# Natural-order casts with parity copies, and Ln and Exp in two pieces, in a strided sparse attention with a rational MLP

## What is computed

```python
scores = scale * np.matmul(q, k.transpose(0, 1, 3, 2))
mask_local = (rel >= 0) & (rel < stride)
mask_strided = (rel >= 0) & (pos[None, :] % stride == pos[:, None] % stride)
...
attn = attn / (np.sum(attn, axis=-1, keepdims=True) + 1e-09)
...
h = x @ w_in
P = a[0] + a[1] * h + a[2] * h2 + a[3] * h3
Q = 1.0 + np.abs(b[0]) * np.abs(h) + np.abs(b[1]) * h2
g = P / (Q + 1e-06)
return (g @ w_out).astype(np.float32)
```

## Time and profile before

| what | value |
|---|---|
| three runs, median (lowest to highest) | 556.41 us (552.62 to 563.49) |
| the profiled execution, its own time | 551.65 us |
| its span, first to last instruction | 549.87 us |
| busy: TensorE, VectorE, ScalarE, POOL | 353.3, 345.4, 255.2, 95.9 us |
| DMA packets, bytes | 176,959, 60.35 MB |

### The profile page before, as it was taken

The page is one execution under the profiler, slowest core; times in us unless marked ns, Lnnn a source line. Parts: engine busy times, 40 slices in busy tenths (PEclk is TensorE's granted clock), DMA queues, the critical chain, the costliest instruction groups (busy, mean ns, idle before and its releaser), DMA issues.

```text
span 549.9 us, 7027 instructions
## 1 busy us (share of the span) xinstructions
PE 353.3 (64%) x2993; PEld 162.9 (30%) x3040; DVE 345.4 (63%) x286; ACT 255.2 (46%) x249; POOL 95.9 (17%) x104
## 2 busy tenths in 40 slices
PE   0010123355662996898479677999998769988763
PEld 0000112113221442444134333344443323333221
DVE  2000013012885795899449758799998996999920
ACT  0010001021735473666707516768847865788500
POOL 9400000050041061514301600010020110100100
PEclk9999999995955797998859967999999989999888
DMA  9999992799299999999994986442261211010101
GB/s 133 119 91 101 184 137 58 131 176 92 46 164 160 160 164 186 194 185 175 186 121 88 161 163 138 87 104 63 61 139 31 60 62 39 38 39 19 57 29 49
DMA packets 176959, 60.35 MB, mean 110 GB/s; under 512 B 164384, under 2 KB 173600, under 8 KB 176416
## 3 DMA queue, kind: packets, MB, share of 16 engines
q1 hardware_dynamic: 133088, 32.11, 40.9%
q0 software_dynamic: 43840, 27.79, 37.5%
HBM read 42.83 MB, written 25.95 MB: 125 GB/s over the span
## 4 chain that ended last, share of the span: by engine, by line
DVE 31%; PE 22%; DMA 16%; SPq 14%; ACT 10%; issue 5%; POOL 0%; DVEq 0%; POOLq 0%
PE ps_h L649 10%; DMA ptL<-pL 8%; PE ps_out L691 7%; SPq L433 6%; DVE u L668 6%; DVE z L676 4%; DMA xt<-xs 4%; SPq L442 4%; DMA xs<-xS 3%; DVE z L674 3%; DVE h L678 3%; ACT u L671 3%; DVE u L666 3%; ACT u L669 3%; DVE z L664 3%
## 5 line engine op out<-in xcount | busy, mean ns | idle before, releaser
L691 PE MATMUL ps_out<-Wout,h 128*128 128x512 bf16 x557 | 144.0, 410 | 24.5 <-ACT os L696 19.3
L649 PE MATMUL ps_h<-xt,Win 128*128 128x512 bf16 x548 | 137.7, 396 | 27.1 <-DMA xt<-xs 12.7
L653 ACT ACTIVATE h<-ps_h 128x512 bf16<-128x512 f32 x144 | 84.9, 597 | 79.8 <-PE ps_h L649 79.8
L691 PEld LDWEIGHTS ps_out<-Wout,h 128*128 128x128 bf16 x576 | 57.0, 104 | 101.5 <-ACT os L696 23.2
L649 PEld LDWEIGHTS ps_h<-xt,Win 128*128 128x128 bf16 x576 | 50.7, 101 | 96.5 <-ACT h L653 32.2
L702 POOL DMA_DIRECT2D out_dram<-os x36 | 37.1, 1121 | 241.1 <-ACT os L696 230.5
L669 ACT ACTIVATE u<-u,consts 128x4096 bf16<-128x4096 bf16 x18 | 66.7, 3706 | 17.2 <-DVE u L668 17.0
L389 POOL DMA_DIRECT2D lq<-in_q_dram x16 | 37.4, 2381 | 206.4 <-DMA vL<-v 205.6
L671 ACT ACTIVATE u<-u 128x4096 bf16<-128x4096 bf16 x18 | 65.1, 3619 | 0.0
L696 ACT ACTIVATE os<-ps_out 128x512 f32<-128x512 f32 x36 | 21.5, 597 | 62.3 <-PE ps_out L691 62.2
L389 POOL DMA_DIRECT2D lk<-in_k_dram x16 | 46.7, 3005 | 0.0
(11 more groups left out here) (41 smaller groups left out, 352.7 us busy)
## 6 DMA issues: line engine op xcount, KB each, us to landing
out_dram<-os POOLq DMA_DIRECT2D x36, 256.0 KB, 3.3
v<-in_v_dram POOLq DMA_DIRECT2D x8, 576.0 KB, 12.1
vL<-v SPq DMA_DIRECT2D x32, 96.0 KB, 3.3
lq<-in_q_dram POOLq DMA_DIRECT2D x16, 144.0 KB, 12.1
lk<-in_k_dram POOLq DMA_DIRECT2D x16, 144.0 KB, 13.5
sq<-in_q_dram POOLq DMA_DIRECT2D x8, 288.0 KB, 7.1
sk<-in_k_dram POOLq DMA_DIRECT2D x8, 288.0 KB, 9.6
vS<-v SPq DMA_DIRECT2D x16, 144.0 KB
```

Source lines behind the costliest of these rows:

```text
L649: r = e.matmul(ph.t[:, :], Win[:, kk, f * 128:(f + 1) * 128], xt.t[:, kk, :], start=(kk == 0), stop=(kk == NK1 - 1))
L653: P.op("act", lambda e, f=f, ph=ph, h=h: e.activation(h.t[:, f % G, :], ph.t[:, :], AF.Copy), 0.53, key, r=[ph], w=[h])
L691: r = e.matmul(po.t[:, :], groups[g].t[:, j, m * 128:(m + 1) * 128], Wout[:, kk, :], start=(kk == 0), stop=(kk == NF - 1))
```

## The change

1. Casts: q and k of all heads, and v of the local heads, go as they lie, in five issues of four heads each; nothing writes 128-byte runs any more. vS is cast by POOL straight from v in DRAM.
2. Loads: q and k come through four transposes, each of four heads and 1,152 rows (local first), all with even positions on the lower half of the partitions and odd ones on the upper. For the local heads four copies from SBUF to SBUF bring the odd positions of heads 0 and 1 to the lower half, and the even positions of heads 2 and 3 to the upper half. The halves of a tile have names of their own for the waits.
3. The local steps take heads 0 and 2, then 1 and 3, in the order local, strided, strided, local. A local score is 36 matmuls of 32 queries (one parity) where it was 18 of 64; the query rows of a block of 64 come out with even positions first, and a matmul writes its 96 columns as two interleaved sets of 48.
4. That order of rows holds through xL, xS and xt. The xs store writes runs of 2,048 numbers in that order. The h copy puts the columns back into their natural order as it writes.
5. Ln and Exp are issued in two pieces of 2,048 columns each, Ln, Ln, Exp, Exp, each waiting for the one before.
6. The last chunk's four sums use the attention's two PSUM tiles, four banks, in place of the one-bank ring.
7. Batch 1's casts and Wout wait for batch 0's loads (the last of vL, the local k); the casts of batch b+2 are written down after attention b. Planner: loads' key -700 becomes -20 (batch 0 keeps it), chunk c's becomes 512 c + 1500 (1000 for the first), mlp2's 1900 becomes 2250, some costs are new, and a DMA counts twice when another queue is busy.

```diff
-    R_lqT = ring("lqT", 4, [128, S])
...
+    SC = S // 2
+    SW = HL * SC
+    PRE = 2 * SC
+    QW = 2 * PRE + 2 * SW
+    R_tq = ring("tq", 2, [128, QW])
+    R_tk = ring("tk", 2, [128, QW])
...
+    def planes(j, idx):
+        if j == 0:
+            return PRE + idx * SC, PRE + SW * 2 + idx * SC
+        return idx * SC, PRE + (2 + idx) * SC
...
+        for n in range(2):
+            for s_t, d_t, t in ((q, q16, T_q[b][n]), (k, k16, T_k[b][n])):
+                bulk(s_t, d_t, b, HL * n, HL, H, t, key, after)
+            if n == 0:
+                bulk(v, vs, b, 0, HL, HL, T_v[b], key, after)
+        vS = vS_of[b] = R_vS.next()
+        for x in range(2):
+            P.op("pool", lambda e, x=x: e.dma_start(
+                vS.t[64 * x:64 * x + SB, :, :, :].rearrange("t h g d -> t h (g d)"),
+                bass.AP(tensor=v.tensor, offset=v.offset + ((b * H + HL) * S + 8 * x) * D,
+                        ap=[[16 * D, SB], [S * D, HL], [1, 8 * D]])),
+                1.0, key, w=[vS], dma=0.6, after=after)
...
+                P.op("sp", lambda e, t=t, d_t=d_t, n=n: e.dma_start_transpose(
+                    t.t[:, PRE + n * SW:PRE + n * SW + SW],
+                    d_t[b, HL * n:HL * n + HL, :, :].rearrange("h (c two) d -> (h c) (two d)", two=2)),
+                    1.3, key + 2 * n, r=[dt_], w=[hf], dma=1.5)
...
+                d0 = 0 if x else PRE + 2 * SW
+                s0 = 2 * PRE if x else PRE
+                P.op("sp", lambda e, t=t, x=x, d0=d0, s0=s0: e.dma_start(
+                    t.t[64 * x:64 * x + 64, d0:d0 + PRE], t.t[64 - 64 * x:128 - 64 * x, s0:s0 + PRE]),
+                    0.5, key + 1, r=[halves[t.name][0]], w=[z], dma=0.3)
...
-        for kind, idx in (("L", 0), ("S", 0), ("L", 2), ("S", 2)):
+        for kind, idx in (("L", 0), ("S", 0), ("S", 2), ("L", 1)):
...
+                        for qp in range(2):
+                            p0 = 64 * (jj % 2) + 32 * qp
+                            for j in range(2):
+                                even, odd = planes(j, idx)
+                                off = 64 * j * QW
+                                r = e.matmul(pst[p0:p0 + 32, j, KW * (jj // 2):KW * (jj // 2) + KW].rearrange(
+                                                 "p (c k) -> p k c", k=2),
...
-                bass.AP(tensor=xs, offset=(b * S + par) * 256, ap=[[16 * 256, SB], [2 * 256, NBK], [1, 256]]),
+                bass.AP(tensor=xs, offset=(b * S + 32 * par) * 256, ap=[[64 * 256, SB // 4], [8 * 256, 4], [1, 8 * 256]]),
...
-                P.op("act", lambda e, f=f, ph=ph, h=h: e.activation(h.t[:, f % G, :], ph.t[:, :], AF.Copy),
+                P.op("act", lambda e, f=f, ph=ph, h=h: e.activation(
+                    h.t[:, f % G, :].rearrange("p (j c k) -> p j k c", k=2, c=32),
+                    ph.t[:, :].rearrange("p (j k c) -> p j k c", k=2, c=32), AF.Copy),
...
+            for fn, kw, fx in ((AF.Ln, dict(bias=eps1, scale=1.0), 0.28), (AF.Exp, dict(scale=-1.0), 0.19)):
+                for part in range(2):
+                    up = u.t[:, 4 * part:4 * part + 4, :]
+                    P.op("act", lambda e, up=up, fn=fn, kw=kw: e.activation(up, up, fn, **kw),
+                         0.833 * W / 2000 + fx, key, r=[T_co], m=[u])
...
+        last = [R_ps.next(), R_ps.next()] if c == NCH - 1 else None
...
     casts(0)
     weights_in()
-    casts(1)
-    weights_out()
     nxt = 0
     st = loads(0)
+    casts(1, after=st["ops"])
+    weights_out(st["ops"])
     for b in range(B):
...
+        xl = attention(b, cur)
         if b + 2 < B:
             casts(b + 2, after=st["ops"])
-        xl = attention(b, cur)
         gather(b, xl)
```

More of the change, by code:

```diff
@@ L130, in schedule @@
             if o.dma is not None:
-                dmafree[e] = max(dmafree[e], t + o.dur) + o.dma
+                at = max(dmafree[e], t + o.dur)
+                busy = any(v > at for k, v in dmafree.items() if k != e)
+                dmafree[e] = at + o.dma * (2 if busy else 1)
                 o.fin = dmafree[e] + 2.2
@@ L271, in ring @@
         return Ring([Tile(f"{name}{i}", sb(f"{name}{i}", shape, ty)) for i in range(n)])
[L274 to L278, removed]
+    q16 = nc.dram_tensor("q16", [B, H, S, D], bf)
+    k16 = nc.dram_tensor("k16", [B, H, S, D], bf)
+    vs = nc.dram_tensor("v16", [B, HL, S, D], bf)
     xs = nc.dram_tensor("xs16", [B, S, HL * D], bf)
[L280 to L281 removed]
+    T_q = [[Tile(f"q{b}{n}") for n in "LS"] for b in range(B)]
+    T_k = [[Tile(f"k{b}{n}") for n in "LS"] for b in range(B)]
     T_v = [Tile(f"v{b}") for b in range(B)]
@@ L378, in bass_strided_sparse_attn__then__act_rational_pade_kernel, with bulk @@
         fill(t, t.t[:, :, KW:128], 0.0, -9e5)
+    def bulk(s_t, d_t, b, h0, nh, hd, t, key, after):
+        n = nh * S * D
+        c = 1024
+        P.op("pool", lambda e: e.dma_start(
+            bass.AP(tensor=d_t, offset=(b * hd + h0) * S * D, ap=[[c, n // c], [1, c]]),
+            bass.AP(tensor=s_t.tensor, offset=s_t.offset + (b * H + h0) * S * D, ap=[[c, n // c], [1, c]])),
+            2.75, key, w=[t], dma=1.4 * nh / 4, after=after)
+    vS_of = {}
+    halves = {t.name: [Tile(t.name + n) for n in "LSX"] for t in R_tq.tiles + R_tk.tiles}
@@ L380, in casts @@
+    def planes(j, idx):
+        if j == 0:
+            return PRE + idx * SC, PRE + SW * 2 + idx * SC
+        return idx * SC, PRE + (2 + idx) * SC
     def casts(b, after=()):
         key = b * 576 - 1500 if b > 1 else -1e5 + 3e4 * b
-        T_lqk[b][0].new()
-        T_lqk[b][1].new()
-        T_sqk[b].new()
+        for n in range(2):
+            T_q[b][n].new()
+            T_k[b][n].new()
         T_v[b].new()
[L387 to L401, removed]
-        bulk(q, sq, HL, T_sqk[b])
-        bulk(k, sk, HL, T_sqk[b])
-        bulk(v, vs, 0, T_v[b])
@@ L405, in casts @@
-        local(1)
+        for n in range(2):
+            for s_t, d_t, t in ((q, q16, T_q[b][n]), (k, k16, T_k[b][n])):
[9 more added lines that the diff above has]
+                1.0, key, w=[vS], dma=0.6, after=after)
@@ L690, in mm @@
                         kk = g * G + j
-                        r = e.matmul(po.t[:, :], groups[g].t[:, j, m * 128:(m + 1) * 128], Wout[:, kk, :],
+                        r = e.matmul(pot, groups[g].t[:, j, m * 128:(m + 1) * 128], Wout[:, kk, :],
                                      start=(kk == 0), stop=(kk == NF - 1))
```

100 lines of the change are left out of this document (44 added, 56 removed).

## The result

The changed kernel took 535.5 us, the median of four runs (531.8 to 543.8), beside 557.5 for the kernel before in the same session: a ratio of 0.961 [0.950, 0.973], 4% faster. The forecast was 453, the range 415 to 512. The direction was right; of a gain of some 100 us a fifth came. Some executions of most kernels here, the old one too, come out one to three per cent longer than the others of the same kernel: a ratio leaves these out, a median and a spread do not.

What follows compares the result with a forecast made beforehand. Transfers were taken to hold the kernel before 340 us, VectorE after, with TensorE close behind. Head 76, middle 359, tail 16.5 and 1.8 around the span gave 453 us; range 415 to 512.

Steps and rivals of the forecast that it cites:

- with the small pieces gone I go by the fullest slices: Middle: transfers would run near the fullest slices' 194 GB/s; at 190 the feed takes 250 us, within VectorE's time.
- POOL's order: Middle: casts of batch b+2 come after attention b and wait for vS's buffer, with stores behind them; cost 0.
- rival 1: Middle: DMA still limits, VectorE at 0.77 until about 300 us; 485 us in all, chance 0.17.
- Net some 70 us: DMA queues: engine time taken away by the change after the added parity copies, out of 431 us.
- Head: Start to VectorE's first MLP operation: 139.15 us falls to 76, with bounds of 60 and 110.
- I take the 0.91: Middle: VectorE's busy rate under the planner's new order, giving 359 us; 0.95 or 0.88 would give 344 or 371.
- Rival 6: Whole kernel: the planner's new order only shifts the waits and time stays within 2%; chance 0.02.
- the pieces' price: ScalarE: second pieces of Ln and Exp add 7.5 us, offset by shorter waits of copies; taken as zero.
- POOL's stores: POOL's queue: output stores might wait behind casts needing a vS buffer; 581 us, chance 0.03.
- rival 3: TensorE: local scores don't overlap, 110 us more work; 513 us in all, chance 0.07.
- Tail: After VectorE's end: 24.2 us falls to 16.5, half of each output sum being done before the last group.
- The h copy: ScalarE: writing columns in steps of two costs 0; at twice the time it would be 86 us.

## Why the prediction was wrong

**Middle: the step "with the small pieces gone I go by the fullest slices" failed.** I priced the casts by what they move, took the fullest slice's 194 GB/s for the rate, and concluded that a feed of 250 us is hidden and VectorE runs at 0.91. The GB/s of the slices, before and after:

```profile
GB/s 133 119 91 101 184 137 58 131 176 92 46 164 160 160 164 186 194 185 175 186 121 88 161 163 138 87 104 63 61 139 31 60 62 39 38 39 19 57 29 49
```
```profile
GB/s 149 198 155 153 159 119 127 165 152 166 151 100 123 104 147 182 147 122 170 166 129 162 146 101 102 151 86 117 50 40 104 47 40 39 39 41 20 60 20 59
```

A slice of 198 stands in the new kernel too, and its early middle moved 140, with VectorE at 0.69. What held VectorE there is for a good part when single transposes land, because TensorE's and VectorE's lists are fixed: the waits behind ptL and for the gather are 52 of its 66.5 idle us. Cutting the casts gave 57 us and the 0.91 that I took; pacing the same bytes gave 23 in the same order; another order gave 15 to 19. How much of the rest is plain volume stays open. The waits for ptL in the earlier trace rows were there to be read: I took 9.2 us of it out of the head as if it went by itself. And "POOL's order", at nothing in the sum, was where the bursts come from: a batch's seven casts are issued at once when vL lands.

The outcome is nearest to rival 1 (485 us, chance 0.17): DMA limits, VectorE slow in the early part. But that rival had the sum of the bytes as its mechanism, at 0.77 until 300. Of a transpose waiting behind casts the prediction spoke only beside the Trainium skill (DMA: Bandwidth & Descriptors, Queues, rings and completion order), by which an engine finishes a whole packet of one queue before it turns to another's. The transposes that landed 20 us after issue amid a burst agree with that, and so does the run with shorter packets in its waits (39.2 us for 55.1), not clearly in its time.

Two terms of the engines' work were off without moving the time. "Net some 70 us" left out that the same bytes still cost some 26 as bulk casts (4.7 of 37.6 parts of 206); measured are 63 off queue 0 and 33 off queue 1 (35.8% of 535.4 for 225), 96 in all. And the transposes didn't grow by a quarter: they have 4,608 rows a batch before and after.

**Head: every step was too short.** First score 33.3 for 22, four steps 34 (to 67.5) for 26, to the first MLP matmul 28.5 for 16, from there to the first group 20.7 for 12. The first is Win's, beside the first transposes: with it moved the score came at 22.6. The second is that of batch 1's casts and Wout beside ptS (14.34 us for the issue of two): with these back in their old place the four steps took 22. I said that what is put back costs nothing because it is wanted late; it was put among steps 2 to 4. The other two go by the lists, and the trace shows where, though no run tests it: SP issues batch 1's loads between the xs store (67.5) and the transposes that bring xS back (87.4), and 12 of VectorE's operations, batch 1's attention, stand ahead of the first group. I had taken ptL's wait out of that stretch, and 4.4 us of it were still there (at 104.5). VectorE's first MLP operation is for the same reason a poor mark of a shorter head: moved 22 to 27 us ahead, it brought nothing at the end in three runs.

**Due times: "I take the 0.91" for any order.** I allowed 344 to 371 us of middle, 27 us between the ends. The order that came with splitting Ln and Exp alone costs 15 to 19 us, one due time 59. Rival 6 had the planner shifting waits to no effect; its effect was larger than most terms of the sum.

**Right.** Queue 0's packets; VectorE's work and its late rate; the pieces' price; POOL's stores, behind which nothing waited. The local scores: 36 matmuls take 0.59 us late in the run where 18 took 0.40, with 0.99 in the first steps, so rival 3 falls. The Trainium skill (SBUF: State Buffer, Door 1: The DMA port swizzle) has non-contiguous PSUM access slow matmuls significantly. No slowing that would cost this kernel is seen, 16 ns each for 22; but the new ones have half the queries, and no run has them writing straight, so the price of the step of two itself stays open.

**Tail: near, by two errors.** It came to 19.1 for 16.5. The 32 matmuls took 7.1 us where I had 8.9, with the copies 1.73 us apart among them; from the last copy's start to the end it took 12.0 us where I had 7.6. The store is issued 0.9 us after that copy in both kernels; what the 4.4 us more at the end are isn't shown:

```profile
516.32 7.08 PE L717 MATMUL ps_s<-Wout,h 128*128 128x512 bf16 x32 [0.78 <-DVE h L702]
518.26 0.60 ACT L722 ACTIVATE os<-ps_s 128x512 f32<-128x512 f32 x1 [7.53 <-PE ps_s L717]
...
523.44 0.60 ACT L722 ACTIVATE os<-ps_s 128x512 f32<-128x512 f32 x1 [1.13 <-PE ps_s L717]
```

**The h copy.** Its zero was off by 0.148 us a copy, and cost 2 to 3 us by the medians, if anything, since ScalarE had room.

## What to carry to other kernels

When transfers are made cheaper, ask not only whether the sum of bytes still limits, but which small transfer a fixed instruction list stands on, and what is issued just ahead of it; a burst that is cheap in all can cost its whole landing time at that point, and spreading it over the steps of the work gave part of that back here without a byte less. A change in an instruction's cost or due time that reorders static lists is a change of its own: hold the order fixed in one run and the instruction in the other before crediting either. A first operation that comes earlier isn't yet a shorter start: see in the lists whether work was only moved past other work.

## What the runs showed of the hardware that I had not expected

- A ScalarE copy of 128x512 from PSUM that writes bf16 in steps of two took 745 ns, and 599 straight, with equal shapes.
- A transpose of the local probabilities landed 20.4 to 20.6 us after its issue amid 1.7 MB of casts, at a median of 4.7 us and a DMA share of 0.85 over the stretch.
- 36 matmuls of 32 queries and 96 columns whose writes step by two took 0.59 us, 16 ns each, while a single one lasts 283 ns by the trace; 18 of 64 queries with straight writes took 0.40, 22 ns each, at 203 ns for a single one.
- With shorter packets (15,296 on queue 0 for 10,176, the same bytes) TensorE's waits for these transposes were 39.2 us for 55.1.
